# A fused convolution and two-layer MLP on one Trainium2 core: a quarter of layer 2's wide down product in three float32r parts

## The chip, the core and the metric

The kernel runs on one core of one Trainium2 chip. That core has a matrix engine (TensorE, PE in the profile; its weight loads are listed apart as PEld), a vector engine (VectorE, DVE), an activation engine (ScalarE, ACT), a general engine (GpSimd, POOL), and a queue engine (SyncE, SP) that only issues transfers. SBUF is the on-chip working memory, PSUM the banks that the matrix engine writes, HBM the memory off the core. The metric is the device time of one execution in microseconds (us), the median of the runs.

## The reference

```python
w = softmax(weight, axis=-1)                   # 8 heads x 7 taps
x = causal_conv(x, w)                          # 2 sequences x 4096 tokens, 192 features, 24 per head
h = x @ w_in;  g = h * sigmoid(1.702 * h)      # layer 1: 192 -> 2048
x = g @ w_out                                  #          2048 -> 192
h = x @ w_in2                                  # layer 2: 192 -> 2048
g = (a0 + a1 h + a2 h^2 + a3 h^3) / (1 + |b0| |h| + |b1| h^2 + 1e-6)
y = g @ w_out2                                 #          2048 -> 192
```

Everything is float32, 8192 tokens in all.

## The kernel before

Tokens go in 16 tiles of 512. Features lie across the partitions, tokens along the free axis, so that the 192 features are a wide part `a` of 128 and a narrow part `b` of 64. The 2048 inner features of a layer are 16 units of 128, taken in pairs ("duos"): 8 duos per tile, 128 duos per layer in all (`TOTAL`). Time goes in steps n = 8 i + s, with i the tile and s = 0 to 7. In step n every engine works on duo n of layer 1 and on some earlier duo of layer 2: its up product on duo n - 10 (`LAG_UP2`), the ratio on n - 11 (`LAG_RATIO`), the down product on n - 12 (`LAG_DOWN2`) or n - 13. Steps 10 to 127 hold both layers ("the stretch with both layers"); the steps from 128 on have only layer 2 ("the tail").

The order is written out by hand: each engine's block has a `step` function, and semaphores join them. Nothing is reordered at run time.

A product at float32 precision is done in one of two ways. Either both operands are float32 (the matrix engine then makes two passes, which the profile shows as two weight loads and two matmul records), or both are split into a high and a low part in float32r and three matmuls are summed: high x high, low x high, high x low. Layer 1's wide down product (`down_a_parts`, L399) uses parts: `g_nhi` is the negated high part of the gelu output, made by ACT (L688), and `g_low` is the low part. `g_low` is made by two transfers: SP copies `g` into `g_low` (L333), and then POOL issues a transfer that adds `g_nhi` to it on the way (L1078, an accumulating transfer). Each is 256 KB, one per unit, so a step has two copies and two adding transfers. Layer 2's wide down product (`down_a`, L392) and the narrow ones of both layers (L414) use float32.

PE's order in a step (L521): transposes of x or y if there are any; layer 1's up product of duo n (L363 to L366); layer 2's up product of duo n - 10 (same lines); the rest of both (L390); then the down products. In an even step these are the narrow ones of two duos of both layers in turn (L416) and layer 1's wide one of duo n - 1 (L409 to L411); in an odd step they are layer 2's wide one of two duos, n - 13 and n - 12 (L396, four float32 matmuls), and layer 1's wide one of duo n - 1.

ACT's order: L662, L679, L681 (read layer 2's product), L686 (gelu), L688 (`g_nhi`), in some steps a copy out of PSUM (L692 at s = 4, L696 at s = 0), L709 and L710 (squares of `m`), L715 (`seed`), small copies. POOL's: L1072 (`m = q * seed`), then the two adding transfers of L1078. SP's: two copies of L333, at s = 1 a store of the whole y tile (L337), at s = 6 four moves of the narrow part of x (L342), at s = 3 the load of a later x tile.

## Time and profile before

| | us |
|---|---|
| median of 3 runs | 1295.6 (1294.58 to 1297.28) |
| the profiled execution: device time | 1295.82 |
| the profiled execution: span on the core | 1294.0 |
| busy in the span: PE / DVE / ACT / POOL | 1268.9 / 1120.2 / 1093.3 / 532.5 |
| granted TensorE clock, mean over the span | 0.997 |
| adding transfers `g_low<-g_nhi`: count, median issue to landing | 236, 4.2 |
| copies `g_low<-g`: count, median issue to landing | 236, 2.4 |

The span runs from the first instruction on the core to the last, and the device time is 1.8 us more. The busy time of PE counts the overlapping records of matmuls once, and their ends are modelled; the start of a weight load is a better mark of where PE is, since the load of a matmul starts when the one before it starts to stream. "Issue to landing" is the time from the issue of a transfer to the last of its semaphore updates.

### The profile page before, as it was taken

How to read it: one execution, taken by the hardware profiler on the slowest of the kernel's cores; microseconds unless marked ns; L12 is line 12 of the kernel's file. 1: busy time of each engine (PE TensorE's matmuls, PEld its weight loads, DVE VectorE, ACT ScalarE, POOL GpSimd, SP SyncE). 2: the span in 40 equal slices, each digit the busy share in tenths (PEclk: the TensorE clock that was granted, in tenths of full speed). 3: DMA queues.
4: the chain of work that ended last, by engine and by line, in shares of the span. 5: the costliest groups of instructions: out<-in, count | busy, mean ns of one | idle time of the engine just before them, and what ended most of it. 6: DMA issues, size and time to landing. Idle time of an engine off the chain costs nothing.

```text
span 1294.0 us, 15433 instructions
## 1 busy us (share of the span) xinstructions
PE 1268.9 (98%) x5102; PEld 755.7 (58%) x5102; DVE 1120.2 (87%) x1230; ACT 1093.3 (84%) x1256; POOL 532.5 (41%) x383
## 2 busy tenths in 40 slices
PE   8999999999999999999999999999999999999986
PEld 6655665655656656566565565665655656556432
DVE  5678998979889897988989798897989989877897
ACT  6678888888988888888888888888888888888775
POOL 2324444444434444444444443443444434444221
PEclk9999999999999999999999999999999999999999
DMA  8235454555555544555545455454545554544100
GB/s 187 86 94 116 119 130 117 126 122 127 123 121 129 126 116 122 131 120 126 121 123 137 108 138 123 120 127 113 138 111 122 135 125 114 120 113 119 25 0 25
DMA packets 107824, 148.62 MB, mean 115 GB/s; under 512 B 20961, under 2 KB 45281, under 8 KB 107745
## 3 DMA queue, kind: packets, MB, share of 16 engines
q0 software_dynamic: 33984, 61.88, 28.1%
q1 hardware_dynamic: 73284, 85.75, 19.7%
q8 instruction: 41, 0.67, 0.2%
q14 instruction: 38, 0.31, 0.1%
q10 hardware_dynamic: 477, 0.01, 0.0%
HBM read 13.64 MB, written 6.29 MB: 15 GB/s over the span
## 4 chain that ended last, share of the span: by engine, by line
PE 93%; DVE 3%; ACT 2%; issue 1%; POOL 1%; DVEq 0%; POOLq 0%; ACTq 0%
PE acc_b L416 17%; PE acc_a L396 16%; PE h L363 9%; PE h L365 9%; PE h L364 9%; PE h L366 9%; PE h L390 7%; PE acc_a L409 6%; PE acc_a L411 5%; PE acc_a L410 4%; POOL work L1072 1%; PE acc_b L422 1%; DVE g L946 1%; PE turned L429 1%; DVE x_in L941 0%
## 5 line engine op out<-in xcount | busy, mean ns | idle before, releaser
L1072 POOL TENSOR_TENSOR work<-work 128x1024 f32<-128x1024 f32 x123 | 295.8, 2405 | 498.5 <-ACT work L681 435.5
L1078 POOL DMA_DIRECT2D g_low<-g_nhi x236 | 208.2, 1018 | 181.0 <-DMA g_low<-g 173.4
L913 DVE TENSOR_TENSOR work<-work,h 128x1024 f32<-128x1024 f32 x128 | 156.2, 1220 | 117.9 <-ACT work L681 117.6
L416 PE MATMUL acc_b<-g,down 128*64 128x512 f32 x512 | 235.3, 601 | 10.1 <-DVE g L946 10.1
L396 PE MATMUL acc_a<-g,down 128*128 128x512 f32 x512 | 238.8, 607 | 0.0
L416 PE MATMUL acc_b<-g,down_b 128*64 128x512 f32 x480 | 218.8, 598 | 0.0
L662 ACT ACTIVATE work<-h,par 128x1024 f32<-128x1024 f32 x128 | 142.7, 1115 | 89.9 <-PE h L390 83.1
L363 PE MATMUL h<-x_a_hi,up_a_hi 128*128 128x512 f32 x510 | 205.3, 403 | 5.2 <-DVE work L915 2.4
L365 PE MATMUL h<-x_a_hi,up_a_lo 128*128 128x512 f32 x510 | 199.2, 391 | 0.0
L364 PE MATMUL h<-x_a_lo,up_a_hi 128*128 128x512 f32 x510 | 199.1, 390 | 0.0
L366 PE MATMUL h<-x_b,up_b_hi 128*128 128x512 f32 x510 | 198.8, 390 | 0.0
L709 ACT ACTIVATE work<-work 128x1024 f32<-128x1024 f32 x127 | 134.8, 1062 | 66.2 <-POOL work L1072 65.0
L915 DVE SCALAR_TENSOR_TENSOR work<-work,par,h 128x1024 f32<-128x1024 f32 x128 | 163.9, 1281 | 4.5
L396 PEld LDWEIGHTS acc_a<-g,down 128*128 128x128 f32 x512 | 91.9, 190 | 120.1 <-issue 104.8
L946 DVE SCALAR_TENSOR_TENSOR g<-work 128x1024 f32<-128x1024 f32 x117 | 143.4, 1226 | 10.6
L916 DVE SCALAR_TENSOR_TENSOR work<-work 128x1024 f32<-128x1024 f32 x124 | 151.4, 1221 | 0.0
L960 DVE SCALAR_TENSOR_TENSOR work<-work,par 128x1024 f32<-128x1024 f32 x117 | 149.7, 1279 | 1.1 <-ACT work L715 1.1
L416 PEld LDWEIGHTS acc_b<-g,down 128*64 128x64 f32 x512 | 64.6, 136 | 143.6 <-issue 129.5
L941 DVE SCALAR_TENSOR_TENSOR work<-work 128x1024 f32<-128x1024 f32 x117 | 142.7, 1220 | 0.4 <-ACT work L709 0.3
L686 ACT ACTIVATE g<-h 128x1024 f32<-128x1024 f32 x128 | 132.6, 1036 | 12.2 <-PE h L390 7.6
L688 ACT ACTIVATE g_nhi<-g 128x1024 fp32r<-128x1024 f32 x128 | 136.0, 1063 | 4.1
L409 PE MATMUL acc_a<-g_nhi,down_nhi 128*128 128x512 f32 x256 | 131.8, 515 | 1.9 <-DMA g_low<-g_nhi 1.5
(141 smaller groups left out, 1964.4 us busy)
## 6 DMA issues: line engine op xcount, KB each, us to landing
g_low<-g SPq DMA_DIRECT2D x236, 256.0 KB, 2.4
g_low<-g_nhi POOLq DMA_DIRECT2D x236, 256.0 KB, 4.2
out<-y_out SPq DMA_DIRECT2D x15, 384.0 KB, 3.0
x_in<-in_x SPq DMA_DIRECT2D x16, 256.0 KB, 3.2
x_in<-in_x SPq DMA_DIRECT2D x32, 64.0 KB, 2.8
work<-in_moe_w_in SPq DMA_DIRECT2D x8, 256.0 KB, 4.7
work<-in_moe_w_in SPq DMA_DIRECT2D x16, 128.0 KB, 4.8
x_b<-x_hb SPq DMA_DIRECT2D x30, 64.0 KB, 2.1
```

Source lines behind the costliest of these rows:

```text
L363: mm(h, l.up_a_hi[:, cols], l.x_a_hi[:, p, :], start=True, stop=False)
L364: mm(h, l.up_a_hi[:, cols], l.x_a_lo[:, p, :], start=False, stop=False)
L365: mm(h, l.up_a_lo[:, cols], l.x_a_hi[:, p, :], start=False, stop=False)
L366: mm(h, l.up_b_hi[:, cols], l.x_b[:, p, :], start=False, stop=False)
L396: done = mm(L2.acc_a[:], L2.down[:, f, 0:P], L2.g[:, v % 3, k, :], start=f == 0, stop=f == STEPS - 1)
L409: mm(acc, down_nhi[:, f, :], g_nhi[:, slot, k, :], start=f == 0, stop=False)
L416: return mm(acc_b[l.acc_row:l.acc_row + DB, :], l.down_b[:, f, :], l.g[:, slot, k, :], start=f == 0, stop=f == STEPS - 1)
L913: tt(tu, tu, h, ALU.mult).then_inc(t2_ready, 1)
L915: stt(tu, tu, par[:, 1:2], h, ALU.add, ALU.mult).then_inc(t3_ready, 1)
L946: stt(gv, s2, d2, zv, ALU.add, ALU.mult).then_inc(g2_ready, 1)
L1072: tt(m, sq_of(v), seed, ALU.mult).then_inc(m_ready, 1)
L1078: pool.dma_start(g_low[:, n % 2, k, :], g_nhi[:, n % 2, k, :], accum_op=ALU.add)\
```

## The change

The second unit of every four of layer 2 (unit 1 of each even duo, `in_parts`) is multiplied in three float32r matmuls in the wide down product, in place of one float32 matmul. This holds for the even duos 0 to 118, which are 60 of the 128; the last eight duos stay as they were. For it ACT makes `g2_nhi` (128 x 512) in the even steps, SP issues a third copy behind layer 1's two, and POOL a third adding transfer behind layer 1's two. PE does the three matmuls at the end of the odd step that follows. The four weight units that this needs are loaded apart and split once, in step 9.

To make room in SBUF, several buffers are shared or cut: `m` now lies in `seed`'s place, so POOL's L1072 also waits for `z1_ready` (DVE's reading of `seed`) in every step, and ACT's L715 waits for its own squares of the step (`s2_ready`); the parts of the narrow x lie in layer 2's `x_b`, with waits that keep them apart; the halo has three slots; `y_out` holds half a tile. y leaves in two stores per tile, at s = 0 and s = 1, each ahead of layer 1's copies of its step in SP's order, where there was one store at s = 1 behind them. For the last eight duos the float32 form of the split units is loaded once more into `conv_a`, from step 120 on.

```diff
+        def in_parts(v):
+            return live(v) and v % 2 == 0 and v < TOTAL - DUOS
...
-                    sp.dma_start(l.down[:, units, :], rows).then_inc(done, 16)
+                    sp.dma_start(down2_a[:, 3 * c:3 * c + 1, :], rows[:, 0:1, 0:P]).then_inc(done, 16)
+                    sp.dma_start(down2_a[:, 3 * c + 1:3 * c + 3, :], rows[:, 2:4, 0:P]).then_inc(done, 16)
+                    sp.dma_start(stage_down2[:, c, :], rows[:, 1, 0:P]).then_inc(done, 16)
+                    sp.dma_start(l.down_b[:, units, :], rows[:, :, P:D]).then_inc(done, 16)
...
+                if s in S_YT and 0 <= i - 3 < TILES - 1:
+                    half = S_YT.index(s)
+                    dst = out_rows[bass.ds((i - 3) * NT, NT), :].rearrange("(j p) d -> p j d", p=P)
+                    sp.wait_ge(y_ready, 4 * (i - 3) + 2 * (half + 1))
+                    sp.dma_start(dst[:, half::2, :], y_out[:]).then_inc(y_stored, 16)
...
-                if s == S_YT[1] and 0 <= i - 3 < TILES - 1:
-                    dst = out_rows[bass.ds((i - 3) * NT, NT), :].rearrange("(j p) d -> p j d", p=P)
-                    sp.wait_ge(y_ready, 4 * (i - 2))
-                    sp.dma_start(dst, y_out[:]).then_inc(y_stored, 16)
+                w = n - LAG_DOWN2
+                if in_parts(w):
+                    sp.wait_ge(g2_ready, w + 1)
+                    wait(sp, g2_p_used, w // 2)
+                    sp.dma_start(g2_low[:].bitcast(F32), L2.g[:, w % 3, 1, :]).then_inc(g2_copied, 16)
+                if n == TOTAL - DUOS:
+                    sp.wait_ge(x1_a_hi_done, TILES)
+                    sp.wait_ge(x1_a_lo_done, TILES)
+                    sp.dma_start(down2_raw, w_out2.rearrange("(c u p) d -> p c u d", u=CU, p=P)[:, :, 1, 0:P])\
+                        .then_inc(down2_again, 16)
                 if s == S_X1_MOVE and tile_live(i + 1):
-                    for done, part, first in ((x1_hb_done, x1_hb, 0), (x1_lb_done, x1_lb, DB)):
+                    high, low = x1_b_parts(i + 1)
+                    for done, part, first in ((x1_hb_done, high, 0), (x1_lb_done, low, DB)):
                         sp.wait_ge(done, i + 1)
...
-                for k in range(2):
+                for k in range(1 if in_parts(v) else 2):
                     f = 2 * (v % DUOS) + k
-                    done = mm(L2.acc_a[:], L2.down[:, f, 0:P], L2.g[:, v % 3, k, :], start=f == 0, stop=f == STEPS - 1)
+                    unit = down2_a[:, 3 * (f // CU) + max(f % CU - 1, 0), :]
+                    if f % CU == 1:
+                        unit = down2_raw[:, f // CU, :]
+                        pe.wait_ge(down2_again, 16)
+                    done = mm(L2.acc_a[:], unit, L2.g[:, v % 3, k, :], start=f == 0, stop=last(v) and k == 1)
                 return done
+            def down_a_parts2(v):
+                c = v % DUOS // 2
+                if v == 0:
+                    pe.wait_ge(d2_hi, 1)
+                    pe.wait_ge(d2_nlo, 1)
+                pe.wait_ge(g2_nhi_ready, v // 2 + 1)
+                pe.wait_ge(g2_low_ready, 16 * (v // 2 + 1))
+                mm(L2.acc_a[:], down2_nhi[:, c, :], g2_nhi[:], start=False, stop=False)
+                mm(L2.acc_a[:], down2_nlo[:, c, :], g2_nhi[:], start=False, stop=False)
+                mm(L2.acc_a[:], down2_hi[:, c, :], g2_low[:], start=False, stop=v % DUOS == DUOS - 2 and v < TOTAL - DUOS)\
+                    .then_inc(g2_p_used, 1)
...
+                if in_parts(n - LAG_DOWN2 - 1):
+                    down_a_parts2(n - LAG_DOWN2 - 1)
...
+                if in_parts(n - LAG_DOWN2):
+                    w = n - LAG_DOWN2
+                    act.wait_ge(g2_ready, w + 1)
+                    wait(act, g2_p_used, w // 2)
+                    fn(g2_nhi[:], L2.g[:, w % 3, 1, :], ACT.Copy, scale=-1.0).then_inc(g2_nhi_ready, 1)
...
                     wait(act, z1_ready, k)
                     wait(act, m_ready, k)
+                    wait(act, s2_ready, k)
                     fn(seed.bitcast(I32), sq_of(k).bitcast(I32), ACT.Copy, scale=-1.0, bias=SEED_BITS)\
                         .then_inc(seed_ready, 1)
...
+                    if i * DUOS + s == LAG_UP2 - 1:
+                        act.wait_ge(down2_loaded, 64 * CHUNKS)
+                        fn(down2_nhi[:], stage_down2, ACT.Copy, scale=-1.0).then_inc(d2_nhi, 1)
+                        fn(down2_hi[:], stage_down2, ACT.Copy).then_inc(d2_hi, 1)
...
+                    if in_parts(v - 3):
+                        dve.wait_ge(g2_p_used, (v - 3) // 2 + 1)
...
                     if live(v + 1):
                         pool.wait_ge(h2_read, v + 2)
-                    if alone(n):
-                        pool.wait_ge(z1_ready, v + 1)
+                    pool.wait_ge(z1_ready, v + 1)
                     wait(pool, s2_ready, v)
                     tt(m, sq_of(v), seed, ALU.mult).then_inc(m_ready, 1)
...
+                w = n - LAG_DOWN2
+                if in_parts(w):
+                    pool.wait_ge(g2_nhi_ready, w // 2 + 1)
+                    pool.wait_ge(g2_copied, 16 * (w // 2 + 1))
+                    pool.dma_start(g2_low[:], g2_nhi[:], accum_op=ALU.add).then_inc(g2_low_ready, 16)
```

Order of instructions. PE, the end of an odd step with s = 1 (duo 48 of layer 1, duos 36 and 37 of layer 2; `acc_a2` and `acc_a1` are the wide sums of layers 2 and 1), before:

```order
L396 MATMUL acc_a2<-g2,down2 128x512 [waits g2_ready]
L396 MATMUL acc_a2<-g2,down2 128x512
L396 MATMUL acc_a2<-g2,down2 128x512 [waits g2_ready]
L396 MATMUL acc_a2<-g2,down2 128x512
L409 MATMUL acc_a1<-g_nhi,down_nhi 128x512 [waits g1_low_0,x2_lo_done,x2_hi_done]
L410 MATMUL acc_a1<-g_nhi,down_nlo 128x512
L411 MATMUL acc_a1<-g_low,down_hi 128x512
L409 MATMUL acc_a1<-g_nhi,down_nhi 128x512 [waits g1_low_1]
L410 MATMUL acc_a1<-g_nhi,down_nlo 128x512
L411 MATMUL acc_a1<-g_low,down_hi 128x512
L363 MATMUL h1<-x_a_hi1,up_a_hi1 128x512 [waits g1_ready]
```

and in the changed kernel:

```order
L440 MATMUL acc_a2<-g2,down2_a 128x512 [waits g2_ready] x2
L440 MATMUL acc_a2<-g2,down2_a 128x512
L466 MATMUL acc_a1<-g_nhi,down_nhi 128x512 [waits g1_low_0,x2_lo_done,x2_hi_done]
L467 MATMUL acc_a1<-g_nhi,down_nlo 128x512
L468 MATMUL acc_a1<-g_low,down_hi 128x512
L466 MATMUL acc_a1<-g_nhi,down_nhi 128x512 [waits g1_low_1]
L467 MATMUL acc_a1<-g_nhi,down_nlo 128x512
L468 MATMUL acc_a1<-g_low,down_hi 128x512
L451 MATMUL acc_a2<-g2_nhi,down2_nhi 128x512 [waits g2_low_ready,g2_nhi_ready]
L452 MATMUL acc_a2<-g2_nhi,down2_nlo 128x512
L453 MATMUL acc_a2<-g2_low,down2_hi 128x512
L403 MATMUL h1<-x_a_hi1,up_a_hi1 128x512 [waits g1_ready]
```

One float32 matmul of layer 2 is gone (its two records of the profile are one row here), and three float32r ones stand at the end of the step, behind layer 1's six, with waits of their own for `g2_nhi` and `g2_low`.

POOL, two steps, an even one first (`m` is the TENSOR_TENSOR), before:

```order
L1072 TENSOR_TENSOR work<-work 128x1024 [waits s2_ready,h2_read,seed_ready]
L1078 DMA g_low<-g_nhi 128x512 [waits g1_copied_0,g1_nhi_ready]
L1078 DMA g_low<-g_nhi 128x512 [waits g1_copied_1]
L1072 TENSOR_TENSOR work<-work 128x1024 [waits s2_ready,h2_read,seed_ready]
L1078 DMA g_low<-g_nhi 128x512 [waits g1_copied_2,g1_nhi_ready]
L1078 DMA g_low<-g_nhi 128x512 [waits g1_copied_3]
```

and in the changed kernel:

```order
L1150 TENSOR_TENSOR work<-work 128x1024 [waits z1_ready,s2_ready,h2_read,seed_ready]
L1156 DMA g_low<-g_nhi 128x512 [waits g1_copied_0,g1_nhi_ready]
L1156 DMA g_low<-g_nhi 128x512 [waits g1_copied_1]
L1162 DMA g2_low<-g2_nhi 128x512 [waits g2_copied,g2_nhi_ready]
L1150 TENSOR_TENSOR work<-work 128x1024 [waits z1_ready,s2_ready,h2_read,seed_ready]
L1156 DMA g_low<-g_nhi 128x512 [waits g1_copied_2,g1_nhi_ready]
L1156 DMA g_low<-g_nhi 128x512 [waits g1_copied_3]
```

In an even step the third adding transfer stands behind the two of layer 1, and the multiplication of the next step behind it.

SP, steps with s = 7, 0, 1 and 2, before:

```order
L333 DMA g_low<-g1 128x512 [waits g1_ready]
L333 DMA g_low<-g1 128x512
L333 DMA g_low<-g1 128x512 [waits g1_ready]
L333 DMA g_low<-g1 128x512
L333 DMA g_low<-g1 128x512 [waits g1_ready]
L333 DMA g_low<-g1 128x512
L337 DMA out_0<-y_out 128x4x192 [waits y_ready]
L333 DMA g_low<-g1 128x512 [waits g1_ready]
L333 DMA g_low<-g1 128x512
```

and in the changed kernel:

```order
L365 DMA g_low<-g1 128x512 [waits g1_ready]
L365 DMA g_low<-g1 128x512
L361 DMA out_0<-y_out 128x2x192 [waits y_ready]
L365 DMA g_low<-g1 128x512 [waits g1_ready]
L365 DMA g_low<-g1 128x512
L370 DMA g2_low<-g2 128x512 [waits g2_p_used,g2_ready]
L361 DMA out_0<-y_out 128x2x192 [waits y_ready]
L365 DMA g_low<-g1 128x512 [waits g1_ready]
L365 DMA g_low<-g1 128x512
L365 DMA g_low<-g1 128x512 [waits g1_ready]
L365 DMA g_low<-g1 128x512
L370 DMA g2_low<-g2 128x512 [waits g2_p_used,g2_ready]
```

The store is cut in two and stands ahead of the copies of its step; the third copy is issued behind layer 1's two in the even steps.

## Rows read from the trace of the kernel before

**Rows 1.** The page: busy us, share of the span, instructions.

```profile
PE 1268.9 (98%) x5102; PEld 755.7 (58%) x5102; DVE 1120.2 (87%) x1230; ACT 1093.3 (84%) x1256; POOL 532.5 (41%) x383
```

**Rows 2.** Windows: engines' busy us, clock, DMA share, GB/s; one tile, one pair of adding transfers.

```profile
446.70:523.30 76.60, 76.60 (x317) 46.27 (x317) 68.28 (x75) 67.15 (x77) 33.43 (x25) 1.00 0.52 124
460.50:463.30 2.80, 2.80 (x10) 1.19 (x10) 2.80 (x4) 1.84 (x3) 0.21 (x1) 1.00 1.04 178
```

**Rows 3.** Weight loads in order, step 51 (start us, us, what).

```profile
462.08 0.19 PEld L396 LDWEIGHTS acc_a<-g,down 128*128 128x128 f32 x1 [0.24 <-issue]
...
464.65 0.19 PEld L409 LDWEIGHTS acc_a<-g_nhi,down_nhi 128*128 128x128 f32 x1 [0.24 <-issue]
...
465.54 0.19 PEld L409 LDWEIGHTS acc_a<-g_nhi,down_nhi 128*128 128x128 f32 x1
...
466.24 0.19 PEld L363 LDWEIGHTS h<-x_a_hi,up_a_hi 128*128 128x128 f32 x1
```

**Rows 4.** Adding transfers of step 50: the first, then the second.

```profile
DMA to landing us min/median/max: 3.4/3.4/3.4
...
L1078 POOL DMA_DIRECT2D g_low<-g_nhi x1: 1178/1178/1178, 459.5 to 459.5; - x1
...
DMA to landing us min/median/max: 4.3/4.3/4.3
```

**Rows 5.** SP and POOL in step 50, in order of time.

```profile
456.11 1.11 SPq L333 DMA_DIRECT2D g_low<-g  x2
...
455.30 2.43 POOL L1072 TENSOR_TENSOR work<-work 128x1024 f32<-128x1024 f32 x1 [3.96 <-ACT work L681]
458.95 1.76 POOL L1078 DMA_DIRECT2D g_low<-g_nhi  x2 [1.22 <-DMA g_low<-g]
```

**Rows 6.** First and last of 58 even steps: load of layer 1's second unit.

```profile
102.06 0.19 PEld L409 LDWEIGHTS acc_a<-g_nhi,down_nhi 128*128 128x128 f32 x1
...
1191.96 0.19 PEld L409 LDWEIGHTS acc_a<-g_nhi,down_nhi 128*128 128x128 f32 x1
```

**Rows 7.** Step 122: first copy; load of layer 1's second unit.

```profile
DMA to landing us min/median/max: 4.0/4.0/4.0
...
1154.43 0.19 PEld L409 LDWEIGHTS acc_a<-g_nhi,down_nhi 128*128 128x128 f32 x1
```

**Rows 8.** Waits: who waited for whom, us in total, times, longest.

```profile
POOL work L1072 <- ACT work L681: 447.1, 105, 8.0
...
PEld acc_a L409 <- DMA g_low<-g_nhi: 5.8, 9, 1.4
```

**Rows 9.** Step 70 (s = 6): landing of its two adding transfers, in order.

```profile
DMA to landing us min/median/max: 3.8/3.8/3.8
...
DMA to landing us min/median/max: 4.6/4.6/4.6
```

**Rows 10.** ACT in steps 50 to 53, in order of time.

```profile
455.04 1.04 ACT L686 ACTIVATE g<-h 128x1024 f32<-128x1024 f32 x1
456.11 1.06 ACT L688 ACTIVATE g_nhi<-g 128x1024 fp32r<-128x1024 f32 x1
457.77 1.06 ACT L709 ACTIVATE work<-work 128x1024 f32<-128x1024 f32 x1 [0.59 <-POOL work L1072]
458.74 1.04 ACT L710 ACTIVATE work<-work 128x1024 f32<-128x1024 f32 x1
...
464.50 1.04 ACT L686 ACTIVATE g<-h 128x1024 f32<-128x1024 f32 x1
...
475.86 0.58 ACT L692 ACTIVATE y_a<-acc_a 128x512 f32<-128x512 f32 x1
...
480.46 1.11 ACT L662 ACTIVATE work<-h,par 128x1024 f32<-128x1024 f32 x1 [0.31 <-PE h L390]
```

**Rows 11.** The tail: ACT, then DVE.

```profile
1222.97 1.05 ACT L715 ACTIVATE work<-g 128x1024 int32<-128x1024 int32 x1
...
1224.84 1.28 DVE L960 SCALAR_TENSOR_TENSOR x_in<-work,par 128x1024 f32<-128x1024 f32 x1
```

More of the change, by code:

```diff
@@ L128, in build_program @@
         g_low = sb("g_low", [P, 2, 2, NT], F32R)
-        L2.down = sb("down2", [P, STEPS, D])
-        L2.down_b = L2.down[:, :, P:D]
+        L2.down_b = sb("down2_b", [P, STEPS, DB])
+        down2_a = sb("down2_a", [P, STEPS - CHUNKS, P])
+        down2_hi = sb("down2_hi", [P, CHUNKS, P], F32R)
+        down2_nhi = sb("down2_nhi", [P, CHUNKS, P], F32R)
+        down2_nlo = sb("down2_nlo", [P, CHUNKS, P], F32R)
+        g2_nhi = sb("g2_nhi", [P, NT], F32R)
+        g2_low = sb("g2_low", [P, NT], F32R)
         up_b_lo = sb("up_b_lo", [P, FF], F32R)
@@ L147, in build_program @@
         diagonal = flat[:, 6 * NT * 2:6 * NT * 2 + taps * P].rearrange("p (k d) -> p k d", d=P)
-        sqa, sqb, t1a, t1b, ab, seed, m, s1 = (work[:, k, :, :] for k in range(8))
+        stage_down2 = flat[:, 6 * NT * 2:6 * NT * 2 + CHUNKS * P].rearrange("p (c d) -> p c d", d=P)
+        sqa, sqb, t1a, t1b, ab, seed, s1 = (work[:, k, :, :] for k in range(7))
+        m = seed
         sq, t1 = (sqa, sqb), (t1a, t1b)
@@ L168, in build_program, with x1_b_parts @@
         conv_b = sb("conv_b", [P, HALF])
-        halo_a = sb("halo_a", [P, (TILES + 1) * HALO])
-        halo_b = sb("halo_b", [DB, (TILES + 1) * HALO])
-        x1_hb = sb("x1_hb", [P, HALF], F32R)
-        x1_lb = sb("x1_lb", [P, HALF], F32R)
+        down2_raw = conv_a[:].rearrange("p (c d) -> p c d", d=P)
+        halo_a = sb("halo_a", [P, 3 * HALO])
+        halo_b = sb("halo_b", [DB, 3 * HALO])
+        def x1_b_parts(tile):
+            return L2.x_b[:, (tile - 1) % 2, 0:HALF], L2.x_b[:, (tile - 1) % 2, HALF:NT]
         first_b = L2.h[:, 0, 0:HALF]
@@ L442, in transpose_y @@
                 for j in range(2):
-                    block = half + 2 * j if ending else 2 * half + j
+                    block = half + 2 * j
                     nc.tensor.transpose(bank[:, j * P:(j + 1) * P], y_a[:, block * P:(block + 1) * P], ident[:])
@@ L636, in x1_b_hi @@
                     wait(act, x1_b_moved, 64 * (tile - 1))
-                    fn(x1_hb[:], conv_b[:], ACT.Copy).then_inc(x1_hb_done, 1)
+                    wait(act, h2_ready, DUOS * (tile - 2))
+                    fn(x1_b_parts(tile)[0], conv_b[:], ACT.Copy).then_inc(x1_hb_done, 1)
             def weights_hi(l, c, staged, done):
@@ L739, in step @@
                     act.wait_ge(y_transposed, 2 * tile + half + 1)
-                    wait(act, y_stored, 16 * tile)
-                    if tile < TILES - 1:
-                        fn(y_out[:, 2 * half:2 * half + 2, 0:P],
+                    if tile < TILES - 1 or half == 0:
+                        wait(act, y_stored, 16 * (2 * tile + half))
+                        fn(y_out[:, :, 0:P],
                            turned[:, 0:2 * P].rearrange("p (j d) -> p j d", d=P), ACT.Copy).then_inc(y_ready, 1)
-                        fn(y_out[:, half::2, P:D],
-                           turned[:, 2 * P:3 * P].rearrange("p (j d) -> p j d", d=DB), ACT.Copy).then_inc(y_ready, 1)
-                    elif half == 0:
-                        fn(y_out[:, 0::2, 0:P],
-                           turned[:, 0:2 * P].rearrange("p (j d) -> p j d", d=P), ACT.Copy).then_inc(y_ready, 1)
-                        fn(y_out[:, 0::2, P:D],
+                        fn(y_out[:, :, P:D],
                            turned[:, 2 * P:3 * P].rearrange("p (j d) -> p j d", d=DB), ACT.Copy).then_inc(y_ready, 1)
@@ L801, in conv_ops @@
                 base = NX * tile
-                at = bass.ds((tile + 1) * HALO, HALO)
+                at = bass.ds((2 if tile + 1 == PER_SEQ else (tile + 1) % 2) * HALO, HALO)
                 def front():
@@ L872, in x1_b_lo @@
                     wait(dve, x1_b_moved, 64 * (tile - 1))
-                    tt(x1_lb[:], conv_b[:], x1_hb[:].bitcast(F32), ALU.subtract).then_inc(x1_lb_done, 1)
+                    high, low = x1_b_parts(tile)
+                    tt(low, conv_b[:], high.bitcast(F32), ALU.subtract).then_inc(x1_lb_done, 1)
             def x1_a_lo(tile, p):
```

38 lines of the change are left out of this document (26 added, 12 removed).

## The prediction

> **What bounds the kernel now.** I read the page's totals first: PE is busy for 1268.9 of 1294.0 us, DVE and ACT for less than nine tenths [rows 1]. Then the windows: in one tile of the stretch with both layers PE is busy for 76.60 of 76.60 us at the full clock (1.00, the upper level of 2.4 GHz), DVE for 68.28 and ACT for 67.15 [rows 2]. So PE paces these steps, and what its instructions take off shows in the end, as long as nothing new makes it wait. The next thing to read is how close PE already is to waiting: the list of waits has nine weight loads of layer 1's wide down product that the adding transfer released [rows 8]. These transfers are the second limit, and the change adds to them.
>
> **What PE saves.** The mark of PE's place is the start of its weight loads. Six halves of float32 matmuls take 464.65 - 462.08 = 2.57 us, so one half takes 0.428 and a float32 matmul 0.857. Three float32r matmuls of the wide down product take 466.24 - 465.54 = 0.70 [rows 3]. Each of the 60 units in parts saves 0.157 us. Duos 0 to 114 are multiplied in the odd steps 13 to 127, where PE paces: 58 x 0.157 = 9.1 us. Duos 116 and 118 fall in the tail, where layer 2's elementwise chain paces and not PE: nothing. If no wait came in, the span would be 1294.0 - 9.1 = 1284.9.
>
> **What the third adding transfer costs.** The three new matmuls stand last in the odd step n + 1 and need g2_low, whose adding transfer POOL issues third in step n. Two numbers set the wait.
>
> How late it lands. In step 50 SP issues two copies at 456.11, POOL the adding transfers at 458.95 and 459.5 [rows 4, 5]. They land after 3.4 and 4.3 us, at 462.3 and 463.8: 0.6 us apart at the issue, 1.5 at the landing. The reason stands in the windows: from 460.50 to 463.30 the 16 transfer engines are 1.04 busy [rows 2]. They are full, so a third one lands one such spacing later. Its issue is in time for that: SP's third copy is issued some 1.2 us after the first, and POOL's third issue follows by 4.2 us after SP's first, at 460.3, 2 us ahead of the landing of the first. The bounds are 0.6 (the spacing of issues) and 1.8; for the upper one I add to 1.5 a part of the time in which a copy holds the engines. I take 1.49, since the engines are full.
>
> When PE wants it. In step 51 the load of layer 1's second unit starts at 465.54, that is 1.7 us after its transfer landed (463.8). I followed this distance, call it the slack, down the timeline for the 58 even steps 12 to 126 (first and last load in [rows 6], with 1.1 and 1.8 of slack). In 48 of them it is 1.54 to 2.37, and 1.75 to 1.8 most often; in six it is 1.00 to 1.38; in one 0.16 and in three 0.04. In step 122, one of these three, the first copy took 4.0 us to land, where the median is 2.4, and the load starts at 1154.43 just as its transfer lands [rows 7]. After the change PE comes to this load 0.857 earlier and to the new matmuls 0.70 after it. So PE waits for max(0, 1.49 + 0.157 - slack). The common slack of 1.77 leaves 0.12 us: no wait. The three and the one give 3 x 1.61 + 1.49 = 6.3 us, the six 2.5, some of the rest 0.4: 9.2 us in all. Nothing gives such a wait back, since PE paces before and behind it.
>
> In steps with s = 6 four moves of 64 KB follow the copies in SP's order. There the two transfers land after 3.8 and 4.6 us in place of 3.4 and 4.3 [rows 9]. Behind one more copy (0.6 us of SP) the moves fall more into the adding transfers. I take 0.15 us of wait for each of 14 tiles, 2 us; the bounds are 0 and 0.3, the delay they cause already.
>
> The Trainium skill, "DMA: Bandwidth & Descriptors", section "Anatomy of one DMA — SWDGE (gpsimd) path", fits a transfer of this path with 2.0 us plus its bytes over 436,000 per us. For 256 KB that is an estimate of 2.6 us, of which 0.6 is movement. By it the third would land 0.6 after the second and the common slack would leave a full microsecond. The trace disagrees: 3.4 us for one, and 1.5 us from one landing to the next [rows 4], and the sum goes by the trace.
>
> **The other parts, each with what hides it.** ACT makes g2_nhi, 128 x 512, 60 times. A copy of that size took 0.58 us. It stands behind L688, where ACT sits idle for 0.59 and waits for POOL's m [rows 10]: it fits there. At s = 4 and s = 0 another copy already fills that place; then ACT comes 0.58 late to L662, where it had 0.31 of idle time at s = 5. The gelu of the next step ends 0.3 us later; in step 51 it ended at 465.54 and PE's next up product loaded at 466.24 [rows 3, 10], so 0.7 covers it. L715 now waits for its squares to end: from L686 to L688, which waits in this way, 1.07 us pass, between the two squares 0.97 [rows 10], so 0.1 per step. The idle time before L662 hides it; in the tail DVE wants the seed at 1224.84, and L715 ended at 1224.02 [rows 11]. If the cover were gone, 0.1 x 117 steps would be 12 us. POOL's wait for z1 ends before its old one: of its multiplications 105 are released by ACT L681 [rows 8], which stands in the next step, after DVE is done with the seed. A third issue takes POOL 0.9 us, with 3.96 idle behind [rows 5]. The stores of y: each is issued ahead of layer 1's copies, but y is ready before that step's gelu, so SP doesn't hold them up. In the start, 16 loads in place of 4 add 12 issues of about 0.6 us to SP, which had nothing else to issue until the moves of step 6. In the last eight duos nothing changes but the place of the weights.
>
> **The sum.** 1294.0 - 9.1 + 9.2 + 2.0 = 1296.1 of span, with 1.8 around it 1297.9: I forecast 1298.0, against 1295.6 of the runs shown (the profiled one is 0.2 above their median). A difference under 0.2%, 2.6 us, can't be told from none here. The forecast is thus "no change, with a lean to slower": the saving is real and is lost in waits for g2_low. Its own range is 1294 to 1301, from how many late transfers fall into even steps (four now; two or six are as well possible, 3 us each way).
>
> **The rivals.**
> First, the saving is kept: the third lands 0.6 us behind the second, or close to it. For it speaks that POOL issues it 0.6 behind; against it the full transfer engines. Then only the four late steps wait, 0.74 less their slack each, 2.7 us: 1295.8 - 9.1 + 2.7 = 1289.4. This is what the figure of that page would give.
> Second, slower: the third lands 1.8 us or more behind the second. The place is the end of the odd steps; the price is 1.8 + 0.157 - slack in 46 of the 58, 19.7 us in all; it decides from a spacing of 1.62 on, where the common slack is used up. Other transfers in the same moment (moves, a fetch of instructions, the third copy) speak for it, the regular 1.5 against it. 1295.8 - 9.1 + 19.7 + 2 = 1308.4.
> Third, the late transfers are chance, and fewer fall on even steps: with one in place of four, 1293.
>
> **How the numbers follow.** Forecast 0.42, first rival 0.24, second 0.26, third 0.08. Faster by over 0.2% (below 1293.0): the first rival, half of the third, a little of the forecast: 0.30. Within: 0.36. Slower (above 1298.2): the second and part of the forecast: 0.34. The range of 8 in 10 goes from 1287.5, just below the first rival, to 1307, into the second.
>
> **What would show it.** In the changed profile: float32 halves still 0.43 and parts 0.23 apart, and an odd step's last load gap 0.157 shorter; a third adding transfer that lands 1.4 to 1.6 us behind the second; the list of waits with PE released by DMA g2_low for some 11 us, most of it in a few steps of over 1 us; ACT's L709 with next to no idle time in even steps. The prediction is wrong if that wait is under 4 us (then the first rival) or over 18 (the second), or if PE waits for something else, such as the gelu at s = 5.

## The result, and the profile after

The changed kernel takes 1305.0 us (median of 6 runs, 1304.0 to 1307.2) against 1295.6: 1.007 of the kernel before, with a 95% interval of 1.0059 to 1.008. The forecast was 1298.0, its own range 1294 to 1301, and 8 in 10 was given to 1287.5 to 1307. The change is slower, by 9 us where 2 were expected: the time lies outside the forecast's own range and inside the wide one, between the forecast and the second rival (1308.4). In a second job (e9_again, below) it took 1304.3. The profiled execution is the slowest of the six (1307.2 us, span 1305.4); that of e9_again is the fastest of its five (1303.25, span 1301.5). The two stand on either side of the medians, so both are used below.

The page after, which answers to [rows 1] (busy us, share of the span, instructions), and its row on POOL's queue of adding transfers (packets, MB, share of 16 engines):

```profile
PE 1266.8 (97%) x5162; PEld 763.1 (58%) x5162; DVE 1122.4 (86%) x1231; ACT 1135.0 (87%) x1318; POOL 585.3 (45%) x443
...
q0 software_dynamic: 42624, 77.61, 35.1%
```

The window of one tile, as in [rows 2]:

```profile
450.70:527.30 76.60, 75.17 (x316) 45.65 (x316) 66.96 (x72) 68.05 (x79) 36.85 (x28) 1.00 0.62 147
```

PE is busy for 75.17 of 76.60 us, where it was busy for all of them: in a stretch that PE paces, it now waits. The list of waits says for what (us in total, times, longest); it answers to [rows 8]:

```profile
POOL work L1150 <- ACT work L741: 442.9, 122, 7.3
...
ACT work L722 <- DVE g L1022: 22.2, 37, 0.7
...
PEld acc_a L451 <- issue: 16.6, 31, 1.1
...
PEld acc_a L466 <- DMA g_low<-g_nhi: 14.1, 16, 1.6
...
PE acc_a L451 <- DMA g_low<-g_nhi: 6.0, 14, 0.7
PE acc_a L466 <- DMA g_low<-g_nhi: 5.9, 11, 1.1
```

L451 is the first new multiplication, L466 the first of a unit of layer 1. One wait shows on two engines: the gap before the load of L451 is put down to "issue", though two semaphores are awaited ahead of it, and part of it stands with PE. So single rows of this list can't be summed. I measured the loss another way, from mark to mark.

**Step lengths.** The mark of a step is the last load of the group of four that ends its up products (L430, before L390). The length of a step is the distance to the next mark; each kind of step, s = 0 to 7, has a shortest length that most steps keep when PE waits for nothing: 9.82, 9.13, 9.46, 9.13, 9.46, 9.61, 9.71, 9.50 us. Summed over steps 12 to 126 they make 1090.3 us. Six steps near the ends (15, 16, 117, 118, 125, 126) are shorter than that, by 2.2 us in all, in every kernel; hence the small negative numbers below, and a kernel's waits are 2.2 us more than its sum. What a kernel takes above the shortest lengths, by the kind of step (the odd steps hold the down products, fed by the transfers of the even step before), in us:

```
                     s=1   s=3   s=5   s=7   even   sum   steps 12-126
before               2.7   2.9   1.8   1.9   -0.2   9.1   1099.4
after                6.4   1.8   3.5   5.0    1.0  17.7   1107.9
e9_again (= after)   4.5   2.5   2.7   6.0   -0.3  15.4   1105.7
```

In the kernel before, nearly all of this is the price of float32: its odd steps are 9.32, 9.32, 9.79 and 9.66 long, almost all of them. Taken step by step, the shortest length among the kernels with the float32 unit (before, e4, e5) is 9.9 us more than among those with all four units in parts (after, e9, e1, e2, e3, e6), 0.19 in each step s = 1 or 3 and 0.16 in each s = 5 or 7; the other 1.4 of 9.1 + 2.2 us are waits. In the kernel after all of it is waits, 19.8 us, and in e9_again 17.6. The rest of the difference lies ahead of step 12 (step 12's mark at 90.6 us, before at 88.05) and behind step 126 (106.95 against 106.61 us).

**A step that waits a little and a late one.** Steps 44 and 45 (s = 4, 5); step 45 takes 10.09 us in place of 9.61: SP, then POOL, then PE's loads in order of time (start us, us), and under it the landings of the first and of the third adding transfer.

```profile
403.19 1.29 SPq L365 DMA_DIRECT2D g_low<-g  x2
404.58 0.55 SPq L370 DMA_DIRECT2D g_low<-g  x1
...
406.42 1.76 POOL L1156 DMA_DIRECT2D g_low<-g_nhi  x2 [1.62 <-DMA g_low<-g]
408.15 0.92 POOL L1162 DMA_DIRECT2D g_low<-g_nhi  x1
...
411.47 0.19 PEld L466 LDWEIGHTS acc_a<-g_nhi,down_nhi 128*128 128x128 f32 x1
...
411.94 0.19 PEld L468 LDWEIGHTS acc_a<-g_low,down_hi 128*128 128x128 f32 x1
412.77 0.19 PEld L451 LDWEIGHTS acc_a<-g_nhi,down_nhi 128*128 128x128 f32 x1 [0.64 <-issue]
```

```profile
DMA to landing us min/median/max: 3.4/3.4/3.4
...
DMA to landing us min/median/max: 4.5/4.5/4.5
```

The third is issued at 408.15 and lands at 412.65; the load of L451 could have come at 412.17, 0.23 behind the last, and comes at 412.77. That is the mechanism of the prediction, at work in a step that is not late.

Steps 52 and 53: PE's loads, and then the landings of SP's two copies, of the two adding transfers of layer 1 and of the third.

```profile
484.14 0.30 PEld L430 LDWEIGHTS h<-x_b,up_b_lo 64*128 64x128 f32 x4 [0.35 <-issue]
...
486.63 0.19 PEld L440 LDWEIGHTS acc_a<-g,down_a 128*128 128x128 f32 x1 [0.24 <-issue]
488.05 0.19 PEld L466 LDWEIGHTS acc_a<-g_nhi,down_nhi 128*128 128x128 f32 x1 [1.23 <-DMA g_low<-g_nhi]
...
489.54 0.19 PEld L466 LDWEIGHTS acc_a<-g_nhi,down_nhi 128*128 128x128 f32 x1 [0.95 <-DMA g_low<-g_nhi]
...
490.98 0.19 PEld L451 LDWEIGHTS acc_a<-g_nhi,down_nhi 128*128 128x128 f32 x1 [0.92 <-issue]
...
495.98 0.30 PEld L430 LDWEIGHTS h<-x_b,up_b_lo 64*128 64x128 f32 x4 [0.35 <-issue]
```

```profile
DMA to landing us min/median/max: 4.4/4.5/4.5
...
DMA to landing us min/median/max: 3.4/3.8/4.3
...
DMA to landing us min/median/max: 5.0/5.0/5.0
```

The copies took 4.4 to 4.5 us in place of 2.3 to 2.5. PE waits three times, the step takes 495.98 - 484.14 = 11.84 us in place of 9.61. Each wait is what the last left over: the landings are 1.5 and 1.4 us apart, and three multiplications take 0.70.

**Who is waited for.** From the load before an awaited one to the second load behind it, over the usual length of that stretch, PE loses ahead of L451, that is for g2_low, 11.4 us in the kernel after and 12.2 in e9_again. Ahead of the units of layer 1 it loses 7.7 and 4.9, where the kernel before loses 1.2. In an odd step PE now comes to layer 1's units 0.86 us earlier than before, since the float32 matmul ahead of them is gone.

### The profile page after: what moved, and what is told of

It is laid out like the page before. It is cut to its first block and busy times, and to the rows that moved or that the text cites. A ratio compares the mean times of both kernels' runs of the same rounds, so it can differ in the third digit from the quotient of the medians.

```text
span 1305.4 us, 16250 instructions
## 1 busy us (share of the span) xinstructions
PE 1266.8 (97%) x5162; PEld 763.1 (58%) x5162; DVE 1122.4 (86%) x1231; ACT 1135.0 (87%) x1318; POOL 585.3 (45%) x443
## 5 line engine op out<-in xcount | busy, mean ns | idle before, releaser
L473 PE MATMUL acc_b<-g,down_b 128*64 128x512 f32 x992 | 242.7, 599 | 9.9 <-DVE g L1022 8.2
L722 ACT ACTIVATE work<-h,par 128x1024 f32<-128x1024 f32 x128 | 142.5, 1114 | 66.2 <-PE h L430 42.1
L440 PE MATMUL acc_a<-g,down_a 128*128 128x512 f32 x384 | 184.1, 613 | 0.0
L777 ACT ACTIVATE work<-work 128x1024 f32<-128x1024 f32 x127 | 134.5, 1059 | 49.7 <-POOL work L1150 47.6
L473 PEld LDWEIGHTS acc_b<-g,down_b 128*64 128x64 f32 x992 | 69.2, 136 | 147.6 <-issue 132.8
L784 ACT ACTIVATE work<-work 128x1024 int32<-128x1024 int32 x124 | 131.6, 1061 | 15.8 <-DVE work L990 1.8
L466 PE MATMUL acc_a<-g_nhi,down_nhi 128*128 128x512 f32 x256 | 131.3, 513 | 6.3 <-DMA g_low<-g_nhi 5.9
L741 ACT ACTIVATE work<-h 128x1024 f32<-128x1024 f32 x128 | 131.3, 1026 | 0.0
```

The costliest lines, as they stand in the source:

```text
L440: done = mm(L2.acc_a[:], unit, L2.g[:, v % 3, k, :], start=f == 0, stop=last(v) and k == 1)
L473: return mm(acc_b[l.acc_row:l.acc_row + DB, :], l.down_b[:, f, :], l.g[:, slot, k, :], start=f == 0, stop=f == STEPS - 1)
```

## The experiments

All times are medians beside runs of the kernel before on the same chip in the same job (its median there: 1295.16, 1295.21, 1295.21 and 1295.55 us). The step table for all of them stands behind e12.

**e1_no_third**: the third copy and adding transfer are taken out; the third multiplication reads g2_nhi.

```diff
-                    sp.dma_start(g2_low[:].bitcast(F32), L2.g[:, w % 3, 1, :]).then_inc(g2_copied, 16)
-                    pool.dma_start(g2_low[:], g2_nhi[:], accum_op=ALU.add).then_inc(g2_low_ready, 16)
-                mm(L2.acc_a[:], down2_hi[:, c, :], g2_low[:], start=False, stop=v % DUOS == DUOS - 2 and v < TOTAL - DUOS)\
+                mm(L2.acc_a[:], down2_hi[:, c, :], g2_nhi[:], start=False, stop=v % DUOS == DUOS - 2 and v < TOTAL - DUOS)\
```

> The changed kernel without SP's third copy, POOL's third adding transfer and PE's wait for it; the third of the new matmuls reads g2_nhi in place of g2_low, so the low part of g is left out. ACT's g2_nhi and all other edits stay. Theory W (the loss is PE's wait for transfers, 14.4 us for g2_low and 4.2 us more for layer 1's g_low in the trace of the changed kernel, against 9 us saved): both waits go, so 1295.6 - 9 = 1286.5, between 1285.5 and 1289. Rival A (the elementwise chain, with ACT's 60 new copies and its later seed, sets the pace): the time stays at 1300 to 1305.

Measured: 1290.4 us (1290.1 to 1292.6), 0.9967 [0.9954, 0.998]. Without the transfer the same multiplications make the kernel 4.8 us faster than before, and 14.6 faster than after. Rival A falls. Yet 4 of the expected 9 us are missing. In the step table 2.5 us remain above the shortest lengths (4.7 us of waits), where none were expected: PE meets layer 1's own second transfer 0.86 us earlier, and in steps behind late copies (19, 25, 72, 81: 3.5 us) it now waits for that. Another 0.9 is in the tail (107.5 us, before 106.6).

**e2_transfers_first** and **e3_all_first**: the third copy and adding transfer are issued ahead of layer 1's two (e2, the first diff); and PE multiplies the unit ahead of layer 1's two as well (e3, both). SP's copies are exchanged in the same way.

```diff
+                    pool.dma_start(g2_low[:], g2_nhi[:], accum_op=ALU.add).then_inc(g2_low_ready, 16)
                 if live(n) and n >= LAG_UP2:
...
-                    pool.dma_start(g2_low[:], g2_nhi[:], accum_op=ALU.add).then_inc(g2_low_ready, 16)
```

```diff
+                if in_parts(n - LAG_DOWN2 - 1):
+                    down_a_parts2(n - LAG_DOWN2 - 1)
...
                     down_a_parts(v1, v1 % 2).then_inc(g1_used, 1)
-                if in_parts(n - LAG_DOWN2 - 1):
-                    down_a_parts2(n - LAG_DOWN2 - 1)
```

> The changed kernel with SP's third copy ahead of layer 1's two in the step, and POOL's third adding transfer ahead of layer 1's two. Nothing is left out; PE's order stays, with the new matmuls last. Theory W: g2_low lands some 4 us earlier, so the wait for it (14.4 us) goes; layer 1's second unit is still wanted 0.86 us earlier than in the kernel before, and behind a third transfer of 1.4 us that overlaps the first by little, so 3 to 6 us of waits for g_low stay: 1289 to 1293. Rival B (the 25% more transfers in the even steps delay layer 1's g_low whatever the order): g_low comes 1 to 1.5 us later, and the time stays at 1300 or more.

> As the kernel with the transfers first, and PE also does the three new matmuls ahead of layer 1's six in the odd step. Theory W: layer 1's g_low is now wanted only 0.16 us earlier than in the kernel before, and g2_low has over 1.5 us to spare, so nearly the whole saving shows: 1286.5 to 1289. Rival A: 1300 or more, since the order of PE and the transfers doesn't touch the elementwise chain. Rival B: 1292 to 1298.

Measured: e2 1298.9 us, 1.0027 [1.0017, 1.0037]; e3 1295.1 us, 0.9996 [0.9987, 1.0005]. e2 lies between its two theories. e3 misses theory W (1286.5 to 1289) and falls in the range of rival B (1292 to 1298), which says that the added transfers delay layer 1's g_low in any order. The order matters: 6.1 us and then 3.7 us are won by it alone. PE's wait for g2_low is gone in both (0.1 us or less), but the wait for layer 1's transfers is 12.8 us in e2 and 9.6 in e3, where it was 7.7 in the kernel after. The list of waits of e2:

```profile
PEld acc_a L466 <- DMA g_low<-g_nhi: 26.7, 45, 1.5
```

45 loads of layer 1's units wait for their transfer, where 16 did in the kernel after. In e3 the waits stand in the even steps (6.1 of 7.3 us in the table). Of them 5.7 us are in steps 16, 32, 84 and 118, each behind an odd step whose copies took 4.2 to 4.7 us. There layer 1's second adding transfer took 5.0 to 5.4 us, in late odd steps of the kernel before 4.2 to 4.3; the third copy, now first in the next step, is issued 0.8 to 1.3 us into that step and is under way beside it. That it slows it is read from these rows, not tested apart.

**e4_unused**: everything is transferred and rounded as in the kernel after, but PE multiplies the unit in float32 (with a neighbour's weights) and never reads g2_low.

```diff
-                for k in range(1 if in_parts(v) else 2):
+                for k in range(2):
...
-                if in_parts(n - LAG_DOWN2 - 1):
-                    down_a_parts2(n - LAG_DOWN2 - 1)
```

> The changed kernel with all its transfers and ACT copies, but PE multiplies the unit as one float32 matmul as in the kernel before (with a neighbour's weights in its place) and never reads g2_nhi or g2_low. Theory W: neither the saving nor the wait, so the time of the kernel before, 1295 to 1297. Rival B (the load of the added transfers itself costs, by delaying layer 1's g_low): 1299 to 1303. Rival A: 1300 or more.

Measured: 1296.6 us, 1.0012 [1.0003, 1.0021]; its steps 12 to 126 take 1099.3 us, as before. That is in theory W's range; rivals A and B (1299 or more) fall. The added load on queues, ACT and POOL costs 1.4 us by itself (0.4 to 2.7), next to the 9 of the change. It costs more only when PE is there to wait for it.

**e5_shared**: the kernel before with the two waits that come with one buffer for seed and m.

```diff
+                    wait(act, s2_ready, k)
...
-                    if alone(n):
-                        pool.wait_ge(z1_ready, v + 1)
+                    pool.wait_ge(z1_ready, v + 1)
```

> The kernel before, with only the waits that come with seed and m in one buffer: ACT's seed also waits for the second square of the step before, POOL's product also waits for DVE's z1. No added transfers, no float32r unit. It asks whether sharing the buffer has a price of its own. Theory W (the 11 us over the expected saving are waits for late transfers): 1295 to 1296 us, no change. Rival S (the shared buffer holds up the elementwise chain and the tail): seed starts 0.2 us later in each step and the tail is 0.5 to 1.5 us longer, 1296.0 to 1298.0 us.

Measured: 1295.4 us, 1.0003 [0.9994, 1.0012]. That is in theory W's range, and the tail is 106.6 us, as before. The interval (-0.8 to +1.6 us) leaves room for a small price, but not for the 9.

**e6_no_copy**: e1 without ACT's rounding of the unit.

```diff
-                if in_parts(n - LAG_DOWN2):
+                if n == LAG_DOWN2:
```

> As e1_no_third (no third copy, no third adding transfer), and ScalarE writes the negated rounded part g2_nhi only once instead of 58 times; the three multiplications read that stale tile, so the unit's own values are left out of the result. It asks what the added 0.58 us of ScalarE costs in 58 steps. If it is hidden, as the prediction put it: 1290.0 to 1290.9 us, as e1_no_third (1290.4). If the elementwise chain (ScalarE and VectorE in turn, 9.26 us per step against PE's 9.13 in steps s=1 and s=3) eats the slack of layer 1's transfers: 1287.5 to 1289.5 us, and ScalarE's first operation of a step starts 0.69 us after its banks are full in all steps again.

Measured: 1289.4 us, 0.9956 [0.9942, 0.9969], against e1's 0.9967 [0.9954, 0.998]. The time lies in the range of the second theory, but the intervals overlap: ACT's 0.58 us in 58 steps costs 1 us by the medians and can't be told from nothing. The second sign was wrong: ACT's first operation still starts 0.83, 0.79 and 1.00 us behind the last up product in steps s = 2, 3 and 4. That delay is thus not made by the added copy. At s = 5 and 6 the copy has a share: 1.25 and 1.04 us in e1, 0.94 and 0.73 in e6. The delay at s = 2 is there in every kernel in which PE's short steps take 9.13 us, and in none in which they take 9.32 (before, e4, e5). From s = 1 to s = 2 it slips from 0.69 to 0.83 in a step of 9.13: a round of the elementwise chain through ACT and DVE takes 9.27. The row of waits for it is ACT L722 <- DVE g above; in the kernel before it was (us in total, times, longest):

```profile
ACT work L662 <- DVE g L946: 4.5, 6, 0.9
```

**e7_two_behind** and **e8_two_first**: two of the four units in parts, those whose transfers are issued at s = 0 and s = 2; in e7 with the order of after, in e8 with that of e3. The other two units keep their float32 weights, and the reload for the last eight duos falls away.

```diff
-            return live(v) and v % 2 == 0 and v < TOTAL - DUOS
+            return live(v) and v % DUOS in (4, 6) and v < TOTAL - DUOS
```

> The kernel after, with only two of the four units of layer 2 in parts: those whose transfers are issued in steps s=0 and s=2 (29 units instead of 58, the ones where the third landing usually comes in time, by 0 to 0.05 us late); the other two stay float32 and are loaded like the rest. Saving 29 x 0.157 = 4.6 us. Theory W-slack (the waits are those of the steps in which the third landing is regularly late, s=4 and s=6): waits below 1.5 us, 1291.5 to 1293.0 us. Theory W-rare (much of the waiting is in a few steps whose copies take 4 us instead of 2.3, which had fitted in before's slack): in the trace of the kernel after the steps s=1 lost 6.4 us over their floor, 3.7 more than they saved, steps s=3 gained 1.0: 1296 to 1299 us.

> As e7_two_behind (two units of four in parts, issued in steps s=0 and s=2), and with the order of e3_all_first: the added copy and adding transfer ahead of layer 1's, and PE's three new multiplications ahead of layer 1's six. Theory W: in e3_all_first's trace the steps s=1 and s=3 lost 1.2 and 0.7 us over their floor, 1.5 and 2.2 less than in the kernel before, and its losses of 3 and 2 us lay in steps whose transfers follow the units of s=4 and s=6; without these, 1291.0 to 1293.5 us, below both kernels. Rival: layer 1's two landings are pushed back by the third whatever the step, and the next steps wait for them: 1295 us or more.

Measured: e7 1295.5 us, 1.0005 [0.9996, 1.0014], between the theories; e8 1293.1 us, 0.9985 [0.9976, 0.9994], in the range of theory W. The trace of e7 is the clearest of all. Its steps s = 1 stand at their shortest length, all of them (0.0 us above); its steps s = 3 lose 5.2 us, of which 4.1 are two single steps, 19 and 75. Step 19: PE's loads; then the transfers around the copies of step 18 (window 149.00 to 155.20, 40 slices of 0.155 us: tenths busy, GB/s, then packets, MB and share by queue).

```profile
156.68 0.19 PEld L435 LDWEIGHTS acc_a<-g,down_a 128*128 128x128 f32 x1 [0.24 <-issue]
157.89 0.19 PEld L461 LDWEIGHTS acc_a<-g_nhi,down_nhi 128*128 128x128 f32 x1 [1.03 <-DMA g_low<-g_nhi]
...
159.40 0.19 PEld L461 LDWEIGHTS acc_a<-g_nhi,down_nhi 128*128 128x128 f32 x1 [0.97 <-DMA g_low<-g_nhi]
...
160.85 0.19 PEld L446 LDWEIGHTS acc_a<-g_nhi,down_nhi 128*128 128x128 f32 x1 [0.92 <-issue]
```

```profile
DMA  0000000000005989999999999600000000000000
GB/s 0 0 0 0 0 0 0 0 0 0 0 0 211 370 330 476 370 383 357 357 344 344 396 383 370 225 13 26 26 26 26 26 26 26 26 26 13 0 0 0
...
q1 hardware_dynamic: 432, 0.79, 34.4%
q8 instruction: 1, 0.02, 0.9%
```

The bulk of the three copies is through at 153.0 us. Then 26 GB/s trickle on for 1.6 us, which is about one engine's share of the 344 to 476 before: I read it as one engine of the 16 that is behind the others. The copies land at 153.95 to 155.24, and POOL issues the adding transfers behind them. In the same window stands one packet of 16 KB on queue 8, a fetch of instructions. See the last section.

**e9_again** is the kernel after once more, **e10_two_again** is e8 once more, in one job.

> The kernel after, unchanged, a second time. Its first profile had 7 us in which TensorE's granted clock was 0.50 (from 83.1 us on) where the kernel before had 1.00, which by steps 10 and 11 cost some 2.5 us. If that belongs to the change, it is there again and the time is 1304 to 1306 us. If it came with one execution: a profile without it, its span some 2 us shorter than 1305.4, and the device times of this job at 1302.5 to 1305.5 us; the waits for g2_low and layer 1's second unit sum to 15 to 20 us again.

> e8_two_first unchanged, a second time, beside the kernel after on the same chip. If its gain is real: 1291.5 to 1294.5 us, 0.998 to 0.999 of the kernel before, and at least 9 us below the kernel after. If it was the spread of one job: 1295 us or more.

Measured: 1304.3 us, 1.0073 [1.006, 1.0087], and 1293.15 us, 0.998 [0.9971, 0.9989]. Both results stand, and both are in the range expected. The granted clock from 84 to 88 us (columns as in [rows 2]), in the profile of after:

```profile
84.00:88.00 4.00, 4.00 (x10) 3.13 (x11) 3.86 (x5) 3.35 (x4) 2.77 (x3) 0.50 0.73 221
```

In that of e9_again:

```profile
84.00:88.00 4.00, 4.00 (x15) 3.23 (x15) 3.93 (x4) 3.34 (x4) 2.79 (x3) 0.76 0.70 217
```

In that of the kernel before:

```profile
84.00:88.00 4.00, 3.95 (x18) 2.99 (x18) 3.96 (x4) 3.41 (x5) 2.80 (x3) 1.00 0.70 215
```

PE is given the lower level (0.50, 1.2 GHz) for 6.8 us in the profile of after and for 3.4 in that of e9_again and of e11, and not in the other eleven. Step 12's mark comes 2.5 and 0.8 us later than in the kernel before. PE is idle for some 2 us just ahead (busy for 2.17 of the 4.00 us from 80 to 84), but so it is in the kernel before (2.00 of 4.00), which keeps 1.00. Nor does it belong to the code: e1 to e4 and e6 are the kernel after up to step 12, and their marks of step 12 come at 87.7 to 88.1 us, where before has 88.05. It came in both profiles of the kernel after; what decides it I don't know.

**e11_three_behind** and **e12_three_first**: three of four units in parts, not the one whose transfers share step s = 6 with the moves; with the order of after, and with that of e3.

```diff
-            return live(v) and v % 2 == 0 and v < TOTAL - DUOS
+            return live(v) and v % DUOS in (0, 4, 6) and v < TOTAL - DUOS
```

> The kernel after, with three of the four units of layer 2 in parts: the one whose transfers are issued in steps s=6, together with the four moves of 64 KB, stays float32 (and is loaded like the rest, except in the last tile). It asks about the prediction's smallest term, 0.15 us per step s=6, 2 us in all. In the two traces of the kernel after, the steps s=7 that follow lost 5.0 and 6.0 us over their shortest length, where the kernel before has 1.9 by its dearer multiplications. If it is the third adding transfer beside the moves: the steps s=7 lose 1.9 us again, the others as in the kernel after, and the time is 3 to 4 us below it, 1299.5 to 1301.5 us. Rival L (the lateness is chance and moves on to the other steps): 1302.5 us or more.

> Three units of four in parts (not the one of s=6) and the order of e3_all_first: the added copy and adding transfer ahead of layer 1's, PE's three new multiplications ahead of layer 1's six. Theory W: from the steps of e3_all_first and e8_two_first, the odd steps lose about 1.2 + 0.7 - 0.3 + 1.9 us over their shortest length and the even ones 2 to 4, some 6 to 7.5 us against 9.1 before and 6.2 in e8_two_first: 1292.5 to 1294.5 us. Rival: the unit of s=4 brings its saving of 2 us and no wait: 1290.5 to 1292 us.

Measured: e11 1303.6 us, 1.006 [1.0046, 1.0073]; e12 1292.7 us, 0.9982 [0.9973, 0.9991]. In e11 the steps s = 7 are back at 2.0 us, as expected, so their loss was the third transfer's. But its other odd steps lose more than in the kernel after. Four copies of 4.1 to 4.5 us fall into its even steps 18, 24, 80 and 108, and the steps behind them lose 2.2, 2.3, 1.8 and 1.8 us, as much as the four of the kernel after; three more (57, 59, 105) lose 0.9, 1.1 and 1.6 with copies on time and adding transfers late. So of the 3 to 4 us expected only about 1 shows, and for the time as a whole rival L holds. e12 lies in the range of theory W (1292.5 to 1294.5).

```
                     s=1   s=3   s=5   s=7   even   sum   steps 12-126
e1_no_third          1.4   1.6  -0.6   0.1    0.0   2.5   1092.8
e2_transfers_first   3.0   0.9   1.3   1.7    3.9  10.8   1101.2
e3_all_first         1.2   0.7  -0.3  -0.4    6.1   7.3   1097.7
e4_unused            2.6   2.7   1.5   2.0    0.3   9.1   1099.3
e5_shared            3.5   2.7   1.8   1.9   -0.4   9.5   1099.7
e6_no_copy           1.6   0.5  -0.8   0.7    0.3   2.3   1092.7
e7_two_behind        0.0   5.2   2.0   2.0   -0.4   8.8   1099.1
e8_two_first         0.0   0.2   1.5   2.4    2.1   6.2   1096.4
e10_two_again        0.0   0.5   1.5   2.5    1.9   6.4   1096.7
e11_three_behind     7.1   3.7   2.4   2.0    0.0  15.2   1105.4
e12_three_first      0.2   0.6  -0.2   2.0    1.4   4.0   1094.3
```

e8, e10 and e12 beat both kernels: the kernel before by 2 to 3 us, the changed one by 11 to 12.

## Why the prediction was right and wrong

**The saving: right, and a little low.** 58 x 0.157 = 9.1 us was forecast; the step lengths give 9.9, 0.19 at s = 1 and 3 and 0.16 at s = 5 and 7. After has the same shortest lengths as e1 and e3.

**The mechanism: right, and not the whole.** PE waits for the third adding transfer; take it and its copy out and 14.6 us go (e1). The wait for g2_low is 11.4 and 12.2 us, where "some 11" was the sign to look for. But by the same signs the prediction is wrong "if PE waits for something else", and it does: 7.7 and 4.9 us for layer 1's own transfers.

**The spacing: nearly.** 1.49 us behind the second was forecast; the median over the 58 even steps is 1.37, and eight in ten lie between 1.31 and 1.44. Both bounds, 0.6 and 1.8, were far off. The Trainium skill's fit of this path ("DMA: Bandwidth & Descriptors", "Anatomy of one DMA — SWDGE (gpsimd) path"), of which the prediction made an estimate of 0.6 us for this spacing, doesn't hold for it in this trace either, and the first rival falls with it.

**The common steps: right at s = 0 and 2.** Forecast: a margin of 0.12 and no wait. At s = 2 the third lands 13.76 us behind the mark and is wanted at 13.85; at s = 0 there is half a microsecond. At s = 4 it is 0.08 us late: PE's step before is short, the chain through ACT and DVE (9.27 us a round) can't keep up with 9.13, and the transfers start 0.28 us later than at s = 0.

**The steps s = 6: this is the step of the sum that was mis-sized.** Forecast 0.15 us each, 2.0 in all, with 0.3 as the upper bound. Measured 5.4 and 6.5 us, about 0.4 each, over the bound. The second transfer lands 13.07 us behind the mark where it landed at 12.45. Of these 0.62 us, 0.21 are a later issue (that chain again, and ACT's added copy: see e6), some 0.2 the first transfer, which takes 4.15 us in place of 3.94 beside one copy more and four moves, and the rest the second, 1.4 behind the first in place of 1.1. I had charged the third transfer with the moves' delay as it stood, and not asked what the added work would do to the two ahead of it. e11, without this unit, has no loss there: its 2.0 us are the price of float32.

**The late steps: the number right by chance.** Four were forecast with 6.3 us, behind steps 18, 40, 100 and 122. Four came, behind others: 8.0 us in after (steps 25, 53, 59, 121: 2.24, 2.22, 1.23, 2.31) and 5.9 in e9_again. All other steps s = 1, 3 and 5: forecast 2.9, measured 4.6 and 4.7. The even steps, forecast nothing: 1.8 and 0.5.

**The sum.** Waits, 11.2 us forecast: measured 8.0 + 5.4 + 4.6 + 1.8 = 19.8 in after and 5.9 + 6.5 + 4.7 + 0.5 = 17.6 in e9_again, of which 1.4 were there before. The start took 2.5 and 0.8 us more. Its added loads are hidden, as forecast (e1 to e4 and e6 show no such delay); the lower clock from 83 us on was not in the sum, and its cause is open. The tail took 0.3 more, forecast nothing. 1294.0 - 9.9 + 18.4 + 2.5 + 0.3 = 1305.3 for after, whose span is 1305.4; 1294.0 - 9.9 + 16.2 + 0.8 + 0.3 = 1301.4 for e9_again, whose span is 1301.5.

**ACT, the shared buffer, POOL's wait for z1, the stores: right as to price** (1.4 us for all of them with the transfers in e4; nothing clear of noise in e5 and e6). But "hidden" held only while PE's steps stayed at 9.32 us: what ate the slack of the transfers was that the chain of ACT and DVE takes 9.27 us to a round and PE now asked for 9.13, and at s = 5 and 6 ACT's added copy too. The sign on L709 (now L777) came true, 0.00 to 0.11 us of idle time in even steps, and told nothing of this; the wait that told was L722's for g.

**Rivals.** The second comes closest by number (1308.4), but not by its reason: the median spacing is 1.37 and not 1.62. The third was right in its thought: where the late copies fall decides some microseconds (e7, e11).

**Open.** Why the tail varies between 106.6 us (before, e5) and 108.0 (e3, e12); what makes the clock fall at 83 us; and whether a program whose fetches are moved would lose its late steps, which was not tried.

## What to carry to other kernels

A saving on the pacing engine brings it nearer to every transfer that it already almost met. Before moving work onto a full queue, list the slack step by step, and for the steps with the least of it recompute every landing ahead of the new one, not only the new one's. Put the added transfer and its reader first in their queues rather than last, and convert only the units whose step has slack: half of the units with the new ones first gained 2 us and three quarters 3, all of them in that order gained nothing, and all of them in the other order lost 9.

## What the runs showed of the hardware

**Late copies go with packets of queue 8, by their number TensorE's fetch of instructions.** A step's first copy of layer 1, 256 KB, takes 2.3 us, and in 7 to 13 of the 115 steps over 3, up to 4.8. Over fourteen profiles I tallied the packets of queue 8 that start from 0.5 us before to 2.3 us behind its issue: 135 of 148 late steps have one, and 41 of 1462 others. In the kernel before it is 9 of 9 and 0 of 106. The page of that kernel, queue by queue:

```profile
q8 instruction: 41, 0.67, 0.2%
```

That is 16.4 KB each, one about every 30 us, and 0.9 to 1.7 us long in the trace. PE has 5102 loads and 5102 multiplications; 10204 / 256 = 39.9. The Trainium skill, "Runtime: NRT & Kernel Launch", "Instruction fetch mechanics", says that a sequencer refills in blocks of 16 KiB, 256 instructions, by a queue of its own, at a cost "mostly hidden". Size and number agree with it. By the tally it is not hidden from the transfers that are under way beside it. The Trainium skill, "DMA: Bandwidth & Descriptors", "Why a DMA increments its semaphore by 16 and not by 1", states that the up to 16 engines of a transfer finish independently and that only all of them together complete it. The trickle of 26 GB/s in e7's window agrees with this. It is an association over many steps and not isolated by an experiment. It would explain why the late steps stand at other places in other programs and at nearly the same ones when a program is run again (24, 37, 43, 52, 58, 77, 83, 117 and 120 in both profiles of the kernel after). e4 speaks for it too: it has the transfers of the kernel after and PE's instructions of the kernel before, and all nine late steps of the kernel before (15, 18, 37, 40, 59, 100, 103, 119, 122) are late in it.

**Adding transfers in a row.** In steps without other transfers three of 256 KB land 3.4, 4.9 and 6.25 us behind the first issue (s = 2), and the 16 engines are 0.97 busy while they are under way (465.09 to 469.89 us of the kernel after, to the landing of the third of step 50).
